# Filler products around the routing's counts, and earlier weight splits in the last expert: a fused attention and mixture-of-experts kernel

## The chip, the cores and the metric

The kernel runs on one core of a Trainium2 chip. The metric is the time of one execution in microseconds (us) on the device. For the kernel before it is 452.43 us, the median of three runs (451.61 to 453.1).

## The reference

Three stages follow each other. A linear attention with a decay per channel runs over 16 (batch, head) pairs of 768 steps, head size 48. Its output, 1536 tokens of 384 numbers, goes through a mixture of 8 experts of which each token takes one, then through a dense layer with a hard-swish.

```python
for t in range(S):
    state = alpha[:, :, t, :, None] * state + np.einsum('bhd,bhe->bhde', k[:, :, t], v[:, :, t])
    y[:, :, t] = np.einsum('bhd,bhde->bhe', q[:, :, t], state)
...
expert_idx = np.argmax(x @ w_gate, axis=1)      # one expert per token, at most 384 tokens each
h = np.maximum(np.einsum('ecd,edf->ecf', disp, w1), 0.0)
y = np.einsum('ecf,efd->ecd', h, w2)            # out[i] = gate_w[i] * y[expert, position]
...
h = x @ w_in
g = h * np.clip(h + 3.0, 0.0, 6.0) / 6.0
out = g @ w_out
```

The model size is 384, an expert's hidden size 1024, the dense layer's 2048.

## The kernel before

The five engines run programs of their own and meet at semaphores.

**Attention** goes over 12 tiles of 128 tokens (NT). TensorE makes scores, state update and output of a tile, turns the output of the tile before (`turn_x`, line 1085) and makes its routing logits (`logits`, line 1093). PSUM has 8 banks, which the stages reuse under other names: `turn_bank` is bank 2, `mix_bank` banks 4 and 5, `y_bank` banks 5 to 7.

**Routing.** VectorE picks each token's expert (`choose`, lines 801 to 809, with the one-hot rows at 805). TensorE turns the one-hot rows into ranks (`ranks_before`, `ranks_within`, lines 1101 to 1112) and, once all tiles are in, into counts per expert (line 1151). This goes in four parts of tiles; the last part, `LATE`, is tiles 10 and 11. GpSimd scatters the gated rows of each token to its slot in DRAM (`slots_x`, line 505), from where SyncE reads an expert's rows back (`load_rows`, line 396). For expert 0 TensorE does not wait for the late tiles' scatter: it gathers their rows with placing matrices that VectorE makes (`place_late`, line 843, products at line 1162), and adds the rows that were read back (line 1167). GpSimd scatters the late tiles only after expert 0's rows are in (`rows_in[0]`), and SyncE reads expert 1's rows (`rows_in[1]`) only after the late scatter is complete.

**Experts.** Weights are used as a sum of two roundings to a shorter float, so each product is three (hi by hi, hi by lo, lo by hi). An expert has 8 hidden tiles f. In step f TensorE makes hidden tile f (lines 1182 to 1184) and the output products of tile f - 3 (lines 1203 to 1205; LAG is 3); the last three tiles' output products of an expert run in the next expert's steps 0 to 2. In steps 3, 4 and 6 (`TURN_AT`) it turns the next expert's rows (`turn_rows`, line 1174), ahead of the first of which it waits for `rows_in`. ScalarE and VectorE follow in the same order: the hidden tile's high part (`hid_hi`, ScalarE, line 662) and rest (`hid_lo`, VectorE, line 946), in step 2 the previous expert's output (`output_hi`, line 653, and `output_lo`, line 926; three chunks c), and the next stage's weight, one of four pieces in each of steps 0, 3, 5 and 7 (`SPLIT_AT`; `split_hi`, line 642, and `split_lo`, line 849). A stage s has four pieces: stages 0 to 7 are the experts, stage 8 (E) is the dense layer's input weight, stage 9 (E + 1) its output weight. SyncE loads a piece into `raw` as soon as VectorE has split the one before it in the same place. In the last expert, pieces of stage 8 are split in steps 0, 3, 5 and 7, and the first piece of stage 9 behind step 7, ahead of the last expert's output.

**Dense layer.** It goes over 4 groups of 384 tokens. Its first products (`first_hidden`, line 1182 again) wait for the last expert's output chunks one by one, and then follow the pattern of the experts with 16 hidden tiles per group.

Of the kernel before, what the change touches and what calls it, by code (L numbers as in the profile page):

```python
# [8 lines left out]
BF16 = mybir.dt.bfloat16  # L9
# [7 lines left out]
def build_program(nc, qk, alpha, v, w_gate, w1, w2, w_in, w_out, out, *, cap):  # L17
    _, D, NT, NPAIR, _ = alpha.shape
    DM = v.shape[2]
    KC = DM // P  # L20
    E = w1.shape[0]
# [21 lines left out]
    FE, FM = F // P, F2 // P  # L43
    PW = KC * 512
    NPC = 4
# [9 lines left out]
    with ExitStack() as ctx:  # L55
        def sb(name, shape, dt=F32):
            return ctx.enter_context(nc.sbuf_tensor(name, shape, dt))

        def sem(name):
            return ctx.enter_context(nc.semaphore(name))  # L60

        bank = [ctx.enter_context(nc.psum_tensor(f"bank{n}", [P, 512], F32)) for n in range(8)]
# [35 lines left out]
        def view(cols):  # L98
            a = arena[0]
            arena[0] += cols  # L100
            assert arena[0] <= ARENA
            return base[:, a:a + cols]
# [78 lines left out]
        zrow = view(DM)  # L181
        tri = sb("tri", [P, P], BF16)
        ones = sb("ones", [P, P], BF16)
# [29 lines left out]
        x_copied = sem("x_copied")  # L213
# [43 lines left out]
        hidden_done = sem("hidden_done")  # L257
# [12 lines left out]
        turn_bank, update_bank = bank[2], bank[3]  # L270
# [2 lines left out]
        xT_bank, logit_bank = bank[6], bank[7]  # L273

        rank_at = [update_bank[:, NPAIR * PR:512]] * 3 + [bank[0][:, :]]
        count_bank = bank[2]
        hidden_bank = bank[0:4]
        rows_bank = bank[4]
        y_bank = bank[5:8]

        TURN_AT = (3, 4, 6)
        SPLIT_AT = (0, 3, 5, 7)
        free_bank = [rows_bank, y_bank[1], y_bank[2]]

        def heads(ap, j):
# [250 lines left out]
        def _(act):  # L536
# [98 lines left out]
            def split_hi(s, w, n):  # L635
                if not isinstance(s, int) or s >= 2:
                    if n < 2:
                        act.wait_ge(hidden_done, (s - 1) * FE)
                    else:
                        act.wait_ge(y_done, (s - 1) * KC)  # L640
                act.wait_ge(raw_in[n], (s + 1) * 16)
                act.activation(w_hi[w][:, n, :], raw[:, n, :], ACT.Copy).then_inc(w_hi_ready, 1)  # L642
# [16 lines left out]
            def expert(e, r):  # L659
                for f in range(FE):  # L660
                    act.wait_ge(hidden_done, e * FE + f + 1)
                    act.activation(hid_hi[f % NH][:, 0:EN], hidden_bank[f % NH][:, 0:EN], ACT.Relu)\  # L662
                        .then_inc(hid_hi_ready, 1)
                    if f == LAG - 1 and not (isinstance(e, int) and e == 0):
                        output_hi(e - 1)
                    if f in TURN_AT and not (isinstance(e, int) and e == E - 1):
                        turn_hi(e + 1, 1 - r, TURN_AT.index(f))
                    if f in SPLIT_AT:
                        split_hi(e + 1, 1 - r, SPLIT_AT.index(f))

            expert(0, 0)
            act.wait_ge(more_end, 1)
            n_more, _ = load_more(act)
# [4 lines left out]
                expert(t * 2 + 1, 1)  # L678
            expert(E - 2, 0)
            expert(E - 1, 1)  # L680
            split_hi(E + 1, 1, 0)
            output_hi(E - 1)

            with act.If(n_more > 0):
# [42 lines left out]
        def _(dve):  # L727
            n = [0]
# [118 lines left out]
            def split_lo(s, w, n):  # L847
                dve.wait_ge(w_hi_ready, s * NPC + n + 1)
                dve.tensor_tensor(w_lo[w][:, n, :], raw[:, n, :], w_hi[w][:, n, :].bitcast(F32), ALU.subtract)\  # L849
                    .then_inc(w_lo_ready, 1)  # L850
# [92 lines left out]
            def expert(e, r):  # L943
                for f in range(FE):
                    dve.wait_ge(hid_hi_ready, e * FE + f + 1)
                    dve.scalar_tensor_tensor(out=hid_lo[f % NH][:, 0:EN], in0=hidden_bank[f % NH][:, 0:EN],  # L946
                                             scalar=0.0, in1=hid_hi[f % NH][:, 0:EN].bitcast(F32),
                                             op0=ALU.max, op1=ALU.subtract).then_inc(hid_lo_ready, 1)
                    if f == LAG - 1 and not (isinstance(e, int) and e == 0):
                        output_lo(e - 1)  # L950
                    if f in TURN_AT and not (isinstance(e, int) and e == E - 1):
                        turn_lo(e + 1, 1 - r, TURN_AT.index(f))
                    if f in SPLIT_AT:
                        split_lo(e + 1, 1 - r, SPLIT_AT.index(f))

            expert(0, 0)
# [5 lines left out]
                expert(t * 2 + 1, 1)  # L962
            expert(E - 2, 0)
            expert(E - 1, 1)
            split_lo(E + 1, 1, 0)
            output_lo(E - 1)

            with dve.If(n_more > 0):
                with dve.Fori(0, n_more) as m:
# [14 lines left out]
                    e = which(m)  # L984
# [42 lines left out]
        def _(pe):  # L1027
# [60 lines left out]
            def logits(i):  # L1088
                pe.wait_ge(xT_copied, i + 1)
                if i >= 1:  # L1090
                    pe.wait_ge(lg_copied, i)
                for c in range(KC):
                    last = pe.matmul(logit_bank[:, i * E:(i + 1) * E], xT[i % 2][:, c * P:(c + 1) * P],
                                     wg[:, c * E:(c + 1) * E], start=(c == 0), stop=(c == KC - 1))
                last.then_inc(logits_done, 1)

            def ranks_before(part):

                a, b = PARTS[part]
                for i in range(a):  # L1100
                    pe.matmul(rank_at[part][:, 0:(b - a) * E].rearrange("p (m e) -> p m e", e=E), ones[:, :],
                              onehot[:, i * E:(i + 1) * E].rearrange("p (o e) -> p o e", o=1)
                              .broadcast_to([P, b - a, E]), start=(i == 0), stop=False, skip_group_check=True)

            def ranks_within(part):
                a, b = PARTS[part]
                pe.wait_ge(onehot_ready, part + 1)
                last = pe.matmul(rank_at[part][:, 0:(b - a) * E], tri[:, :], onehot[:, a * E:b * E], start=(part == 0),
                                 stop=(b - a == 1), skip_group_check=True)
                for i in range(a, b - 1):  # L1110
                    c = i + 1
                    last = pe.matmul(rank_at[part][:, (c - a) * E:(b - a) * E].rearrange("p (m e) -> p m e", e=E), ones[:, :],
                                     onehot[:, i * E:(i + 1) * E].rearrange("p (o e) -> p o e", o=1)
                                     .broadcast_to([P, b - c, E]), start=False, stop=(i == b - 2), skip_group_check=True)
                last.then_inc(ranks_done, 1)
# [30 lines left out]
            pe.wait_ge(masked, NT)  # L1146
            ranks_before(3)
            logits(NT - 1)
            ranks_within(3)
            for i in range(NT):  # L1150
                last = pe.matmul(count_bank[:, 0:E], ones[:, :], onehot[:, i * E:(i + 1) * E],
                                 start=(i == 0), stop=(i == NT - 1))
            last.then_inc(counts_ready, 1)

            def gather_first_rows():

# [54 lines left out]
            n_more, _ = load_more(pe)  # L1211
# [158 lines left out]
```

## Time and profile before

| | us |
|---|---|
| median of three runs | 452.43 (451.61 to 453.1) |
| the profiled execution | 450.51 |
| its span, first to last instruction | 448.0 |
| TensorE products busy in it | 420.9 (94%) |
| VectorE busy | 260.6 (58%) |
| ScalarE busy | 210.8 (47%) |
| GpSimd busy | 53.7 (12%) |
| mean granted clock of TensorE | 0.988 |

Times in the rows are from the span's start. Engines are named PE (TensorE products), PEld (its weight loads), DVE (VectorE), ACT (ScalarE), POOL (GpSimd), SPq (SyncE's DMA issues). The granted clock is a share of 2.4 GHz: 1.00 is that, 0.50 is 1.2 GHz. "L1162" is line 1162. Some products in 32-bit floats have two records each, so a count of x12 can stand for 6 products.

### The profile page before, as it was taken

To read this page: it belongs to the slowest core of one execution; us is meant where nothing else is said; L and a number is where in the kernel's file an instruction comes from. 1 tells how busy PE (TensorE), PEld (TensorE's weight loads), DVE (VectorE), ACT (ScalarE), POOL (GpSimd) and SP (SyncE) were. 2 spreads that over 40 slices of the span, in tenths; PEclk is the share of its full clock that TensorE was granted. 3 is DMA by queue.
4 is the path that set the end of the run, shared out by engine and by line. 5 is a ranking of instruction groups with operands and counts; after the bars stand their busy time and mean duration, and the time that the engine had idled before them with its cause. 6 is when DMAs were issued, how large, how long until landed. Compare 5 with 4: busy or idle time off the path is not lost.

```text
span 448.0 us, 8023 instructions
## 1 busy us (share of the span) xinstructions
PE 420.9 (94%) x3111; PEld 414.6 (93%) x3111; DVE 260.6 (58%) x473; ACT 210.8 (47%) x408; POOL 53.7 (12%) x66
## 2 busy tenths in 40 slices
PE   1899999869999999999998999999999999999993
PEld 1799989859999999999998999999999999999993
DVE  7999999857767767767765563243333333143330
ACT  1254677526565565666663643343334333343331
POOL 9000003630000000000003830110002000110002
PEclk9999999969999999999999999999999999999998
DMA  8999951674856856856758000010001000010001
GB/s 168 284 305 300 311 168 55 183 278 141 255 173 207 251 175 209 246 174 214 222 183 301 4 1 0 15 41 0 1 0 55 0 1 0 4 50 1 0 0 53
DMA packets 37922, 56.34 MB, mean 126 GB/s; under 512 B 4768, under 2 KB 27808, under 8 KB 37888
## 3 DMA queue, kind: packets, MB, share of 16 engines
q1 hardware_dynamic: 35840, 50.95, 37.9%
q0 software_dynamic: 1920, 4.73, 2.7%
q8 instruction: 23, 0.38, 0.4%
q10 hardware_dynamic: 128, 0.20, 0.2%
q14 instruction: 11, 0.09, 0.1%
HBM read 44.06 MB, written 11.81 MB: 125 GB/s over the span
## 4 chain that ended last, share of the span: by engine, by line
PE 86%; DVE 7%; issue 2%; ACT 2%; DMA 1%; POOL 1%; SPq 0%; ACTq 0%; DVEq 0%; POOLq 0%
PE bank L1183 12%; PE bank L1184 12%; PE bank L1182 12%; PE bank L1325 7%; PE bank L1324 7%; PE bank L1323 7%; PE bank L1203 5%; PE bank L1205 5%; PE bank L1204 4%; PE bank L1075 3%; PE bank L1034 2%; PE bank L1053 2%; DVE bwd L744 1%; PE bank L1064 1%; DVE arena L757 1%
## 5 line engine op out<-in xcount | busy, mean ns | idle before, releaser
L849 DVE TENSOR_TENSOR w_lo<-raw,w_hi 128x1536 fp32r<-128x1536 f32 x40 | 70.1, 1758 | 23.3 <-ACT w_hi L642 23.2
L1012 DVE SCALAR_TENSOR_TENSOR arena<-arena,bank 128x384 f32<-128x384 f32 x64 | 35.4, 553 | 82.9 <-ACT arena L713 82.9
L713 ACT ACTIVATE arena<-bank,bias 128x384 f32<-128x384 f32 x64 | 37.0, 577 | 67.9 <-PE bank L1184 67.8
L1182 PE MATMUL bank<-x_hi,w_hi 128*128 128x384 f32 x192 | 64.5, 336 | 1.8 <-DVE w_lo L849 1.8
L1183 PE MATMUL bank<-x_lo,w_hi 128*128 128x384 f32 x192 | 65.1, 339 | 0.0
L1324 PE MATMUL bank<-w_lo,hid_hi 128*128 128x384 f32 x192 | 64.8, 337 | 0.0
L1325 PE MATMUL bank<-w_hi,hid_lo 128*128 128x384 f32 x192 | 64.7, 337 | 0.0
L1184 PE MATMUL bank<-x_hi,w_lo 128*128 128x384 f32 x192 | 64.7, 337 | 0.0
L1323 PE MATMUL bank<-w_hi,hid_hi 128*128 128x384 f32 x192 | 64.6, 337 | 0.0
L1016 DVE SCALAR_TENSOR_TENSOR hid_lo<-arena,hid_hi 128x384 fp32r<-128x384 f32 x64 | 35.7, 558 | 37.9 <-ACT hid_hi L716 37.9
L1182 PE MATMUL bank<-xt_hi,w_hi 128*128 128x232 f32 x192 | 54.4, 283 | 0.1
L716 ACT ACTIVATE hid_hi<-arena 128x384 fp32r<-128x384 f32 x64 | 33.6, 525 | 43.1 <-DVE arena L1012 43.1
L1203 PE MATMUL bank<-hid_hi,w_hi 128*128 128x232 f32 x192 | 53.2, 277 | 0.0
L642 ACT ACTIVATE w_hi<-raw 128x1536 fp32r<-128x1536 f32 x36 | 53.2, 1480 | 0.0
L1205 PE MATMUL bank<-hid_lo,w_hi 128*128 128x232 f32 x192 | 52.9, 275 | 0.0
L1184 PE MATMUL bank<-xt_hi,w_lo 128*128 128x232 f32 x192 | 52.8, 275 | 0.0
L1183 PE MATMUL bank<-xt_lo,w_hi 128*128 128x232 f32 x192 | 52.6, 274 | 0.0
L1204 PE MATMUL bank<-hid_hi,w_lo 128*128 128x232 f32 x192 | 52.5, 274 | 0.0
L662 ACT ACTIVATE hid_hi<-bank 128x232 fp32r<-128x232 f32 x64 | 23.0, 364 | 34.9 <-PE bank L1184 34.9
L1182 PEld LDWEIGHTS bank<-x_hi,w_hi 128*128 128x128 f32 x192 | 36.1, 188 | 1.8 <-DVE w_lo L849 1.8
L1203 PEld LDWEIGHTS bank<-hid_hi,w_hi 128*128 128x128 f32 x192 | 36.8, 192 | 0.5 <-DVE hid_lo L946 0.2
L1182 PEld LDWEIGHTS bank<-xt_hi,w_hi 128*128 128x128 f32 x192 | 36.7, 191 | 0.2 <-issue 0.2
(135 smaller groups left out, 776.8 us busy)
## 6 DMA issues: line engine op xcount, KB each, us to landing
raw<-w SPq DMA_DIRECT2D x32, 768.0 KB, 4.8
slots_x<-arena SPq DMA_DIRECT2D x8, 576.0 KB, 6.6
arena<-qk SPq DMA_DIRECT2D x22, 192.0 KB, 4.7
arena<-slots_x SPq DMA_DIRECT2D x8, 384.0 KB, 4.8
raw<-w_in SPq DMA_DIRECT2D x4, 768.0 KB, 4.3
raw<-w_out SPq DMA_DIRECT2D x4, 768.0 KB, 4.7
arena<-alpha SPq DMA_DIRECT2D x24, 96.0 KB, 4.0
arena<-v SPq DMA_DIRECT2D x12, 192.0 KB, 4.9
```

The lines of the kernel that those rows point to most:

```text
L642: act.activation(w_hi[w][:, n, :], raw[:, n, :], ACT.Copy).then_inc(w_hi_ready, 1)
L713: act.activation(shifted[f % 2], hidden_bank[f % NH][:, 0:BR], ACT.Relu, bias=bias3[:, 0:1]).then_inc(shift_ready, 1)
L849: dve.tensor_tensor(w_lo[w][:, n, :], raw[:, n, :], w_hi[w][:, n, :].bitcast(F32), ALU.subtract)\
L1182: pe.matmul(bank_, hi, hi_in, start=(kc == 0), stop=False)
L1183: pe.matmul(bank_, hi, lo_in, start=False, stop=False)
L1184: return pe.matmul(bank_, lo, hi_in, start=False, stop=(kc == KC - 1))
L1203: pe.matmul(bank_, hi, h_hi, start=(f == 0), stop=False)
L1204: pe.matmul(bank_, lo, h_hi, start=False, stop=False)
L1205: last = pe.matmul(bank_, hi, h_lo, start=False, stop=(f == FE - 1))
L1323: pe.matmul(bank_, h_hi, hi, start=(f == 0), stop=False)
L1324: pe.matmul(bank_, h_hi, lo, start=False, stop=False)
L1325: last = pe.matmul(bank_, h_lo, hi, start=False, stop=(f == FM - 1))
```

## The change

There are two parts.

First, around the last ranks and the counts. A new function `keep_busy(n)` issues n products of the `ones` matrix with 384 columns of `zrow` (zeros, read as bfloat16) into `turn_bank`, whose content nothing reads there any more. Seven go behind the last logits, nine behind the counts. The counts go to bank 5 instead of bank 2, and wait for the last copy of x out of that bank.

Second, in the last expert (E - 1) the pieces of stage 8 are split in steps 0, 1, 3 and 5 and the first piece of stage 9 in step 6; none is left behind the steps. `split_hi` waits, for the first two pieces, for the hidden tiles of the expert that used that piece (4 or 8 of them) and not for all 8 tiles of it or of its successor.

```diff
-        count_bank = bank[2]
+        count_bank = bank[5]
...
+        LAST_SPLIT_AT = (0, 1, 3, 5, 6)
...
             def split_hi(s, w, n):
                 if not isinstance(s, int) or s >= 2:
                     if n < 2:
-                        act.wait_ge(hidden_done, (s - 1) * FE)
+                        act.wait_ge(hidden_done, (s - 2) * FE + 4 * (n + 1))
...
-                    if f in SPLIT_AT:
+                    if isinstance(e, int) and e == E - 1:
+                        if f in LAST_SPLIT_AT[:NPC]:
+                            split_hi(E, 0, LAST_SPLIT_AT.index(f))
+                        elif f in LAST_SPLIT_AT:
+                            split_hi(E + 1, 1, 0)
+                    elif f in SPLIT_AT:
                         split_hi(e + 1, 1 - r, SPLIT_AT.index(f))
...
             expert(E - 1, 1)
-            split_hi(E + 1, 1, 0)
             output_hi(E - 1)
...
+            def keep_busy(n):
+
+                for _ in range(n):
+                    pe.matmul(turn_bank[:, 0:DM], ones[:, :], zrow.bitcast(BF16)[:, 0:DM], start=True, stop=True,
+                              skip_group_check=True)
...
             logits(NT - 1)
+            keep_busy(7)
             ranks_within(3)
+            pe.wait_ge(x_copied, NT)
             for i in range(NT):
                 last = pe.matmul(count_bank[:, 0:E], ones[:, :], onehot[:, i * E:(i + 1) * E],
                                  start=(i == 0), stop=(i == NT - 1))
             last.then_inc(counts_ready, 1)
+            keep_busy(9)
```

VectorE's program has the same edit with `split_lo`.

The order on TensorE from the last tile's turn to the end of expert 0's gather, before:

```order
L1085 MATMUL bank<-ident,x_rows 128x128 x3
L1101 MATMUL bank<-onehot,ones 128x16 x10
L1093 MATMUL bank<-arena 128x8 x3
L1108 MATMUL bank<-onehot,tri 128x16
L1112 MATMUL bank<-onehot,ones 128x8
L1151 MATMUL bank<-onehot,ones 128x8 x12
L1162 MATMUL bank<-arena,x_rows 128x256 x6
L1167 MATMUL bank<-ident,arena 128x128 x6
```

and in the changed kernel, whose line numbers are larger:

```order
L1095 MATMUL bank<-ident,x_rows 128x128 x3
L1117 MATMUL bank<-onehot,ones 128x16 x10
L1103 MATMUL bank<-arena 128x8 x3
L1110 MATMUL bank<-arena,ones 128x384 x7
L1124 MATMUL bank<-onehot,tri 128x16
L1128 MATMUL bank<-onehot,ones 128x8
L1169 MATMUL bank<-onehot,ones 128x8 x12
L1110 MATMUL bank<-arena,ones 128x384 x9
L1181 MATMUL bank<-arena,x_rows 128x256 x6
L1186 MATMUL bank<-ident,arena 128x128 x6
```

The rows of line 1110 are the fillers; nothing else moved.

The order on VectorE in the last expert, from its step 3 to the output of it, before (`w_lo` is a split, `x_lo` an output chunk, `hid_lo` a hidden tile):

```order
L946 SCALAR_TENSOR_TENSOR hid_lo_73<-bank,hid_hi_69 128x232
L849 TENSOR_TENSOR w_lo<-raw,w_hi 128x1536
L946 SCALAR_TENSOR_TENSOR hid_lo_70<-bank,hid_hi_66 128x232
L946 SCALAR_TENSOR_TENSOR hid_lo_71<-bank,hid_hi_67 128x232
L849 TENSOR_TENSOR w_lo<-raw,w_hi 128x1536
L946 SCALAR_TENSOR_TENSOR hid_lo_72<-bank,hid_hi_68 128x232
L946 SCALAR_TENSOR_TENSOR hid_lo_73<-bank,hid_hi_69 128x232
L849 TENSOR_TENSOR w_lo<-raw,w_hi 128x1536 x2
L923 TENSOR_LOAD offsets
```

and in the changed kernel:

```order
L952 SCALAR_TENSOR_TENSOR hid_lo_73<-bank,hid_hi_69 128x232
L855 TENSOR_TENSOR w_lo<-raw,w_hi 128x1536
L952 SCALAR_TENSOR_TENSOR hid_lo_70<-bank,hid_hi_66 128x232
L952 SCALAR_TENSOR_TENSOR hid_lo_71<-bank,hid_hi_67 128x232
L855 TENSOR_TENSOR w_lo<-raw,w_hi 128x1536
L952 SCALAR_TENSOR_TENSOR hid_lo_72<-bank,hid_hi_68 128x232
L855 TENSOR_TENSOR w_lo<-raw,w_hi 128x1536
L952 SCALAR_TENSOR_TENSOR hid_lo_73<-bank,hid_hi_69 128x232
L929 TENSOR_LOAD offsets
```

Two splits stood behind the last hidden tile and ahead of the output; now one stands ahead of the last hidden tile. The other went to step 1, between hidden tiles 1 and 2 and so ahead of expert 6's output chunks:

```order
L952 SCALAR_TENSOR_TENSOR hid_lo_70<-bank,hid_hi_66 128x232
L855 TENSOR_TENSOR w_lo<-raw,w_hi 128x1536
L952 SCALAR_TENSOR_TENSOR hid_lo_71<-bank,hid_hi_67 128x232
L855 TENSOR_TENSOR w_lo<-raw,w_hi 128x1536
L952 SCALAR_TENSOR_TENSOR hid_lo_72<-bank,hid_hi_68 128x232
L929 TENSOR_LOAD offsets
```

The second split of this piece is the one that is new there.

## Rows read from the trace of the kernel before

**Rows 1.** Windows: stretch, length, busy us per engine (instructions), clock, DMA share, GB/s
```profile
92.00:92.67 0.67, 0.00 (x0) 0.00 (x0) 0.39 (x3) 0.17 (x1) 0.13 (x1) 1.00 0.05 18
92.67:95.50 2.83, 0.54 (x14) 0.48 (x15) 2.35 (x15) 1.33 (x3) 0.00 (x0) 0.50 0.29 87
95.50:99.50 4.00, 4.00 (x10) 3.19 (x11) 1.51 (x11) 0.00 (x0) 1.27 (x2) 0.50 1.00 359
99.50:101.50 2.00, 2.00 (x16) 1.88 (x14) 0.31 (x1) 0.62 (x2) 0.68 (x1) 1.00 1.01 378
```

**Rows 2.** Timeline, 91 to 100 us: start, length, engine, line, operation, idle before it
```profile
91.13 0.83 PE L1093 MATMUL bank<-arena 128*128 128x8 f32 x6 [0.34 <-ACT arena L574]
...
93.27 0.20 PE L1108 MATMUL bank<-onehot,tri 128*128 128x16 bf16 x1 [1.30 <-DVE onehot L805]
...
93.34 0.46 PE L1151 MATMUL bank<-onehot,ones 128*128 128x8 bf16 x12
...
95.50 4.81 PE L1162 MATMUL bank<-arena,x_rows 128*128 128x256 f32 x12 [1.70 <-DVE arena L843]
```

**Rows 3.** Timeline of POOL and SPq; then DMA issues around 104 us (KB, us to landing)
```profile
97.93 0.97 POOL L505 DMA_INDIRECT slots_x<-arena,slot  x1 [5.80 <-DMA arena<-slots_x]
...
103.69 0.37 SPq L396 DMA_DIRECT2D arena<-slots_x  x1
...
arena<-slots_x SPq DMA_DIRECT2D x1, 384.0 KB, 3.1
```

**Rows 4.** Timeline of PE in expert 0, steps 3 and 4
```profile
106.83 0.40 PE L1174 MATMUL bank<-ident,arena 128*128 128x128 f32 x2
...
108.25 0.38 PE L1203 MATMUL bank<-hid_hi,w_hi 128*128 128x232 f32 x1
```

**Rows 5.** Timeline of SPq, ACT, DVE and PE around expert 7, steps 0 to 3
```profile
205.00 15.12 SPq L331 DMA_DIRECT2D raw<-w_in  x4
221.77 14.45 SPq L331 DMA_DIRECT2D raw<-w_out  x4
...
218.47 1.49 ACT L642 ACTIVATE w_hi<-raw 128x1536 fp32r<-128x1536 f32 x1
220.22 0.37 ACT L662 ACTIVATE hid_hi<-bank 128x232 fp32r<-128x232 f32 x1 [0.27 <-PE bank L1184]
...
222.89 0.88 ACT L653 ACTIVATE x_hi<-bank 128x232 f32 x3 [0.29 <-PE bank L1205]
...
219.99 1.76 DVE L849 TENSOR_TENSOR w_lo<-raw,w_hi 128x1536 fp32r<-128x1536 f32 x1
...
223.40 1.01 DVE L926 TENSOR_TENSOR x_lo<-bank,x_hi 128x232 f32 x3 [0.37 <-ACT x_hi L653]
...
224.05 0.27 PE L1203 MATMUL bank<-hid_hi,w_hi 128*128 128x232 f32 x1
224.16 0.27 PE L1204 MATMUL bank<-hid_hi,w_lo 128*128 128x232 f32 x1
```

**Rows 6.** Timeline at the hand-over to the dense layer, then its window
```profile
234.07 3.43 DVE L849 TENSOR_TENSOR w_lo<-raw,w_hi 128x1536 fp32r<-128x1536 f32 x2 [0.97 <-ACT w_hi L642]
...
235.74 1.04 ACT L653 ACTIVATE x_hi<-bank 128x232 f32 x3 [0.32 <-PE bank L1205]
...
236.01 0.27 PE L1205 MATMUL bank<-hid_lo,w_hi 128*128 128x232 f32 x1
...
237.42 1.01 DVE L926 TENSOR_TENSOR x_lo<-bank,x_hi 128x232 f32 x3
238.04 0.34 PE L1182 MATMUL bank<-x_hi,w_hi 128*128 128x384 f32 x1 [1.75 <-DVE w_lo L849]
238.21 0.34 PE L1183 MATMUL bank<-x_lo,w_hi 128*128 128x384 f32 x1
...
236.20:238.00 1.80, 0.08 (x1) 0.12 (x1) 1.80 (x3) 0.57 (x2) 0.00 (x0) 1.00 0.46 49
```

**Rows 7.** Instructions of line 926: count, ns min/median/max, first and last start
```profile
L926 DVE TENSOR_TENSOR x_lo<-bank,x_hi x6: 387/392/399, 223.4 to 238.0; 128x232 f32 x6
```

More of the change, by code:

```diff
@@ L952, in expert @@
                         turn_lo(e + 1, 1 - r, TURN_AT.index(f))
-                    if f in SPLIT_AT:
+                    if isinstance(e, int) and e == E - 1:
+                        if f in LAST_SPLIT_AT[:NPC]:
+                            split_lo(E, 0, LAST_SPLIT_AT.index(f))
+                        elif f in LAST_SPLIT_AT:
+                            split_lo(E + 1, 1, 0)
+                    elif f in SPLIT_AT:
                         split_lo(e + 1, 1 - r, SPLIT_AT.index(f))
@@ L964, in _ @@
             expert(E - 1, 1)
-            split_lo(E + 1, 1, 0)
             output_lo(E - 1)
```

## The prediction

> **What bounds the kernel now.** I read the windows first. TensorE is busy through nearly all of the span, so it is the bound, and time can only be won where it waits or runs slowly. Two places stand out. [rows 1] show the first: between 92.67 and 99.5 us the granted clock is 0.50 (1.2 GHz), on both sides of it 1.00 (2.4 GHz). Before it fell the engine had been idle since 91.96 us, and in the half-clock stretch it first had 0.54 us of work in 2.83, then 4.00 in 4.00. The timeline of TensorE [rows 2] shows why: after the last logits it waits 1.30 us for the one-hot rows of the last two tiles, and after the counts 1.70 us for VectorE's placing matrices. The gather (line 1162) then takes 4.81 us, nearly all of it at half clock.
>
> The second place is the hand-over from the experts to the dense layer: TensorE starts the last product of expert 7 at 236.01 us and the first dense product at 238.04, with 1.75 us idle between them [rows 6]. VectorE has been in two weight splits since 234.07, and the three output splits that TensorE waits for (line 926) stand behind them and start at 237.42.
>
> The third view to read is what is late next. [rows 3] follow the late tiles through DRAM: GpSimd scatters them from 97.93 us on, as soon as the first rows have landed, SyncE issues the read of expert 1's rows at 103.69, and that read takes 3.1 us to land, so it is there at about 106.79. The first product that needs it is the transpose at 106.83 [rows 4]. TensorE's arrival and the landing now coincide, with no slack worth naming.
>
> **Part 1, the fillers.** 7 products go between the logits and the last ranks, 9 behind the counts. No row has a bfloat16 product of 384 columns; the nearest is the dense product of as many columns, one starting 0.17 us after the other (238.04, 238.21) [rows 6]. A lower bound for each is the 8-column product: twelve in 0.46 us, 0.04 each [rows 2]; an upper one is 0.34, the same at half clock. I take 0.17 because the columns are the same. Then 7 x 0.17 = 1.19 us, from about 91.9 to 93.1, ahead of the one-hot rows at 93.27; and 9 x 0.17 = 1.53 us from about 93.75 to 95.28, ahead of 95.50. At full clock they fit into the two waits and cost nothing. The counts go to another bank, for which the added wait on the last copy of x has long been met: it is the copy that the transposes ahead already waited for.
>
> If they hold the clock, the 4.00 us between 95.5 and 99.5 [rows 1] become 2.00. The gather (95.50 + 4.81 = 100.31 before) ends 2.0 us sooner, at about 98.3. The first rows are needed there and have landed by 97.93, since GpSimd starts on them then [rows 3]. Everything TensorE does up to the transpose moves from 106.83 to 104.83.
>
> There the gain ends. Nothing in the chain scatter, read, landing waits for TensorE: GpSimd waits for a DMA, SyncE for GpSimd's scatter [rows 3]. TensorE will stand before the transpose from 104.83 until 106.79. Of 2.00 us it keeps 106.83 - 106.79 = 0.04. Behind it the 0.17 us delay at 108.25, where VectorE's rest of hidden tile 1 was late (line 1203) [rows 4], goes too, since VectorE catches up while TensorE stands. The sum for part 1 is 0.04 + 0.17 = 0.2 us. The bounds are 0 and 2.0 us, the second if the landing were as early as TensorE. I take 0.2, by the row of the landing itself.
>
> **Part 2, the splits of expert 7.** The dense layer's input weight is split at steps 0, 1, 3, 5 instead of 0, 3, 5, 7, the first piece of its output weight at step 6 instead of behind step 7. The new waits on hidden tiles ask for 4 or 8 tiles of the expert two stages back, which all steps have long passed; in expert 7 the wait of the output piece falls from 64 tiles done to 60, which step 6 satisfies. The data are there: the four input pieces were issued from 205.00 on over 15.12 us and the first output piece at 221.77 [rows 5], 9 us ahead of step 6 at 230.3. SyncE's later loads and the clearing of the output start some 2 to 4 us sooner; no stall of [rows 6] hangs on them, so I cost that at nothing.
>
> *What it takes away.* ScalarE starts the first output copy at 235.74 [rows 6]. Without splits in between, VectorE follows a start of ScalarE's copy by 0.51 us (222.89 to 223.40) [rows 5], its operation takes 0.39 [rows 7], and TensorE starts 0.23 after its end (237.42 + 0.39 = 237.81, start 238.04) [rows 6]. That makes 235.74 + 0.51 + 0.39 + 0.23 = 236.87 instead of 238.04, a gain of 1.17 us.
>
> *What it adds.* A step is 18 products, 0.112 us apart, so 2.01 us. ScalarE splits at step 1 that much after step 0's split (218.47), right behind the hidden tile of 220.22, so from about 220.48 to 221.97. VectorE's half starts at 221.99 and takes 1.76, so hidden tile 2 comes at 223.66 and the first of expert 6's output splits at 223.97 instead of 223.40 [rows 5]. TensorE's product at 224.05 overwrites the bank that this one reads. Before, 223.40 + 0.39 + 0.23 = 224.02, just in time. Now it is 223.97 + 0.62 = 224.59: TensorE waits 0.54 us, and all of expert 7 behind it moves by as much. The next two chunks are in time, as VectorE's spacing ((1.01 - 0.39) / 2 = 0.31) is below TensorE's three products (3 x 0.11) [rows 5].
>
> *The end of it.* With TensorE 0.54 later the step-6 split runs on VectorE until about 234.3, hidden tile 7 until 234.7, and TensorE wants it at 235.6. The net of part 2 is 1.17 - 0.54 = 0.63 us. The bounds are 1.17 (if the 0.54 does not appear) and 0.3 (if a hidden tile also comes late by as much again as a piece's 0.31).
>
> **Sum.** 0.2 + 0.63 = 0.83 us. The profiled execution took 450.51 us (span 448.0 and 2.5 around it), so it would take 449.7. It was 1.9 us below the median of the runs shown, 452.43; taken from that, 451.6 us. A measurement of this kernel can tell about 0.3%, 1.36 us, from no change: faster means below 451.07, slower above 453.79.
>
> **The rivals.**
> *A, the forecast:* most of the clock's gain is swallowed by the landing of expert 1's rows, 0.83 us remain, 451.6 us. Its own range is 451.0 to 452.1. For it speaks that the chain of [rows 3] never touches TensorE. Chance 0.5.
> *B, the gain gets through:* if the late chain lands by 104.8 in an ordinary execution, TensorE keeps 2.0 + 0.17 us, and with part 2 that is 2.8: 449.6 us. Against it: the issue alone is at 103.69 [rows 3], and it would have to be 2 us earlier. Chance 0.13.
> *C, the other executions lose more to the clock:* the half-clock stretch need not start and end at the same place in each. If the kernel before recovers 1 us later than here, it starts the transpose 0.5 us later, and part 1 is worth 0.7; if 2 us later, 1.2. With part 2 that is 1.3 to 1.8 us, 450.9 us in the middle. That the ordinary runs take 1.9 us more than the profiled one leaves room for this. Chance 0.22.
> The Trainium skill, TensorE: Matmul & The Clock Gate, section on the clock gate, says the monitor runs freely and so the same kernel has more or fewer slow products from run to run. By that rule the gain would differ by execution and C would be the rule rather than the exception; one trace cannot show it.
> *D, the fillers do not hold the clock:* the work ahead of 91.96 is sparse too, and the fillers stream zeros. If the clock still falls at 92.67 and recovers at 99.5, the second group takes 9 x 0.34 = 3.1 us from about 94.0 to 97.1, the gather starts 1.6 us late, and by 99.5 it has had 2.4 us at half clock, worth 1.2. Of its 2.0 + 0.81 = 2.81 us at full clock 1.6 remain, so it ends at 101.1 instead of 100.31, 0.8 lost against 0.63 won: 452.6 us. Chance 0.05.
> *E, the new wait lowers the clock (slower):* TensorE would stand about 2.0 us before the transpose. If the clock falls there as it did at 92.67, it may stay down for the 6.8 us of [rows 1], and dense work loses half of that, 3.4 us: 451.6 + 3.4 = 455.0 us. It decides if an idle time of 2.0 us between dense products is enough. Against it: the 1.75 us at 236.2 left the clock at 1.00 [rows 6]. Chance 0.1.
>
> **How the numbers follow.** Faster is B, C's larger part and A's upper edge: 0.13 + 0.18 + 0.04 = 0.35. Slower is E and a little of D: 0.1. Within 0.3% is the rest, 0.55. The range of 449.6 to 453.0 takes in A, B, C and D and leaves out E and some of B.
>
> **What would show it.** The changed kernel's windows should show the clock at 1.00 from 92 to 98 us, the gather near 2.8 us, and then a new idle time of nearly 2 us before line 1174's counterpart, ended by the DMA of the rows. If that idle time is missing, the part on the landing is wrong. In expert 7 a gap of about 0.5 us before the first output product of step 3 and one of about 0.6 us at the hand-over, in place of 1.75, would confirm part 2. A clock of 0.50 after 106 us would be rival E.

## The result and the profile after

The changed kernel takes 455.05 us (median of 6 runs, 454.51 to 460.91), the kernel before 451.7 beside it (6 runs, 451.18 to 453.1). The ratio is 1.0102, 95% interval 1.007 to 1.0133: slower by about 1%, where the prediction said 451.6 us and 0.2% faster. Ratios here leave out executions that were disturbed from outside, so one can differ a little from the ratio of two medians.

| | before | after |
|---|---|---|
| the profiled execution, us | 450.51 | 454.51 |
| its span, us | 448.0 | 452.7 |
| mean granted clock of TensorE | 0.988 | 0.986 |

I go through the after profile in order of time, the routing first. Timeline of TensorE (line 1110 is the fillers, 1181 the gather, 1193 the transposes), then windows (length, busy of PE, PEld, DVE, ACT, POOL, clock, DMA share, GB/s):

```profile
91.53 1.94 PE L1110 MATMUL bank<-arena,ones 128*128 128x384 bf16 x7
...
93.68 2.48 PE L1110 MATMUL bank<-arena,ones 128*128 128x384 bf16 x9
96.00 2.75 PE L1181 MATMUL bank<-arena,x_rows 128*128 128x256 f32 x12
...
105.57 0.44 PE L1193 MATMUL bank<-ident,arena 128*128 128x128 f32 x2
```
```profile
92.00:94.00 2.00, 2.00 (x22) 1.10 (x20) 1.56 (x12) 0.32 (x2) 0.00 (x0) 0.51 0.29 108
94.00:96.00 2.00, 2.00 (x10) 1.07 (x9) 1.80 (x11) 1.02 (x2) 0.00 (x0) 0.64 0.45 115
96.00:98.00 2.00, 2.00 (x11) 1.77 (x11) 0.80 (x5) 0.00 (x0) 0.21 (x1) 1.00 1.06 398
```

The fillers close both waits of [rows 2]. The clock falls all the same in this execution, from 92.0 us on, but is back at 95.5, ahead of the gather, which takes 2.75 us and not 4.81. The transposes start at 105.57, with no wait ahead of them, because the rows were early too: SyncE issued their read sooner than in [rows 3]:

```profile
102.36 0.37 SPq L398 DMA_DIRECT2D arena<-slots_x  x1
```

So up to here 106.83 - 105.57 = 1.26 us are won, more than the 0.2 of the sum. The delay of 0.17 us at line 1203 [rows 4] mostly went too: the same product starts 1.39 us sooner (106.86 against 108.25). Expert 7's step 0 (hidden tile at 218.77, before 220.22 [rows 5]) is 1.45 us ahead.

Expert 7, in the timelines of ACT, PE and DVE (line 664 is a hidden tile, 655 and 932 are the output splits, 1222 to 1224 the output products, 1201 and 1202 dense products):

```profile
218.77 0.36 ACT L664 ACTIVATE hid_hi<-bank 128x232 fp32r<-128x232 f32 x1 [0.27 <-PE bank L1203]
...
222.48 0.28 PE L1203 MATMUL bank<-xt_hi,w_lo 128*128 128x232 f32 x1
223.07 0.34 PE L1222 MATMUL bank<-hid_hi,w_hi 128*128 128x232 f32 x1 [0.31 <-DVE x_lo L932]
...
234.83 1.04 ACT L655 ACTIVATE x_hi<-bank 128x232 f32 x3 [3.07 <-PE bank L1224]
235.34 1.08 DVE L932 TENSOR_TENSOR x_lo<-bank,x_hi 128x232 f32 x3 [2.12 <-ACT x_hi L655]
...
235.10 0.27 PE L1224 MATMUL bank<-hid_lo,w_hi 128*128 128x232 f32 x1
240.25 0.66 PE L1201 MATMUL bank<-x_hi,w_hi 128*128 128x384 f32 x1 [4.88 <-issue]
240.71 0.52 PE L1202 MATMUL bank<-x_lo,w_hi 128*128 128x384 f32 x1
```

The stall of step 3 is there, ended by the output split as forecast: 0.59 us lie between the starts of two products (222.48 and 223.07) that are otherwise 0.11 apart. And VectorE does what it was freed for: it idles 2.12 us and then follows ScalarE's copy by 0.51 us. But TensorE takes no notice. It starts 4.91 us after the first of these splits (240.25 - 235.34), which last 1.08 us together, and its idle time of 4.88 us is put down to "issue": it waited for no semaphore. The chain of work that ended last goes through the same idle time:

```profile
236.43 3.82 issue
240.25 0.66 PE bank L1201
```

The windows of these microseconds, columns as above, answer to the one of [rows 6]:

```profile
236.00:238.00 2.00, 0.00 (x0) 0.00 (x0) 0.42 (x2) 0.00 (x0) 1.05 (x2) 1.00 1.08 404
238.00:240.00 2.00, 0.00 (x0) 0.00 (x0) 0.00 (x0) 0.00 (x0) 1.70 (x2) 0.70 1.05 391
240.00:242.00 2.00, 1.75 (x6) 1.78 (x7) 0.00 (x0) 0.00 (x0) 1.39 (x3) 0.50 0.49 164
242.00:244.00 2.00, 2.00 (x8) 2.00 (x7) 0.00 (x0) 0.00 (x0) 1.69 (x2) 0.50 0.03 1
244.00:246.00 2.00, 2.00 (x9) 2.00 (x8) 0.00 (x0) 0.00 (x0) 1.40 (x2) 0.59 0.02 1
```

Two things are new against [rows 6]. The clock falls in the gap and stays at 0.50 until about 245.6 us. And the DMA engines, at a share of 0.46 and 49 GB/s in the window of [rows 6], are full (1.08, 404 GB/s). What fills them is the clearing of the output, 2304 KB. SyncE's timeline shows when it is issued, behind the last four weight pieces:

```profile
220.32 10.97 SPq L333 DMA_DIRECT2D raw<-w_out  x4
232.34 0.39 SPq L450 DMA_DIRECT2D out<-arena  x1
```

In the kernel before, SyncE's timeline has it at 237.29 us, by when TensorE was about to start:

```profile
237.29 0.39 SPq L448 DMA_DIRECT2D out<-arena  x1
```

Last, the DMA queues of the changed kernel from 237.6 to 237.7 us, within the gap (queue, kind: packets, MB, share), show a packet of instructions; TensorE resumes at 240.25:

```profile
q1 hardware_dynamic: 25, 0.04, 101.6%
q8 instruction: 1, 0.02, 55.4%
```

**The account.** The span grew by 4.7 us. Expert 7 started 1.45 us earlier and grew by 0.54 (step 0's tile to the last output product: 235.10 - 218.77 = 16.33 us, before 236.01 - 220.22 = 15.79). From that product to the first dense one it is 5.15 us instead of 2.03, +3.12. Behind it the dense products come 0.32 us apart instead of 0.17 for 5.35 us, of which (0.32 - 0.17) / 0.32 is lost, +2.5. The sum is -1.45 + 0.54 + 3.12 + 2.5 = 4.7 us.

### The profile page after: what moved, and what is told of

Read it like the earlier page. It is cut to its first block, busy times and chain, and to the rows that moved or that the text cites. A ratio compares the mean times of both kernels' runs of the same rounds, so it can differ in the third digit from the quotient of the medians.

```text
span 452.7 us, 8059 instructions
## 1 busy us (share of the span) xinstructions
PE 425.1 (94%) x3127; PEld 417.1 (92%) x3127; DVE 260.1 (57%) x473; ACT 210.6 (47%) x408; POOL 48.9 (11%) x66
## 4 chain that ended last, share of the span: by engine, by line
PE 73%; DVE 15%; issue 6%; DMA 4%; ACT 1%; POOL 1%; SPq 0%; DVEq 0%; POOLq 0%; ACTq 0%
PE bank L1203 12%; PE bank L1202 12%; PE bank L1201 12%; PE bank L1344 7%; PE bank L1343 7%; PE bank L1342 7%; PE bank L1222 5%; PE bank L1224 5%; PE bank L1223 5%; DVE bwd L750 3%; DVE arena L779 3%; DVE arena L763 3%; DMA arena<-slots_x 1%; PE bank L1193 1%; DVE arena L795 1%
## 5 line engine op out<-in xcount | busy, mean ns | idle before, releaser
L1201 PE MATMUL bank<-x_hi,w_hi 128*128 128x384 f32 x192 | 65.7, 342 | 4.9 <-issue 4.9
L1202 PE MATMUL bank<-x_lo,w_hi 128*128 128x384 f32 x192 | 66.1, 344 | 0.0
L1203 PE MATMUL bank<-x_hi,w_lo 128*128 128x384 f32 x192 | 65.7, 342 | 0.0
```

Of the source, the lines that this page charges most:

```text
L1201: pe.matmul(bank_, hi, hi_in, start=(kc == 0), stop=False)
L1202: pe.matmul(bank_, hi, lo_in, start=False, stop=False)
L1203: return pe.matmul(bank_, lo, hi_in, start=False, stop=(kc == KC - 1))
```

## The experiments

**Theory 1:** the early splits let SyncE issue the clearing 5 us sooner. Between the last output product and the first dense one TensorE jumps over a block of code for overflowing experts (`n_more > 0`), which this input never runs, and must read the instructions behind it through the same DMA engines. Behind the clearing that read takes long. Two rivals stand against it: the order of the splits, that is the computation itself, and the routing's fillers. The expectations number these differently, so each says what its theory 2 or 3 is; theory 1 is the same in all. Every result is against the kernel before on the same chip (451.48, 451.64, 452.07 and 452.29 us in the four groups of runs).

### Each part alone

`fillers_only` is part 1 of the diff on the kernel before, `splits_only` part 2.

> Only part 1, the filler products and the counts' bank; the splits of the last expert as before. Theory 1 (the loss is the clearing of the output, which part 2 issues 5 us earlier and which then holds up TensorE's instruction reads at the hand-over): part 1 is innocent, the time is that of before or 0.2 to 1.5 us below it, and the first dense product comes about 1.75 us after the last expert product, as before. Theory 2 (the fillers do the harm, by running at half clock ahead of the gather or by moving the clock's later state): this kernel has at least half of the loss of 3.35 us, so 453.4 us or more where before has 451.7.

> Only part 2, the earlier splits of the last expert; no fillers. Theory 1: the whole loss is here. The gap at the hand-over is 4 to 5 us, released by nothing that the profile shows, the clock falls behind it, and the time is 4 to 5 us above before (455.5 to 457), more than the full change's 3.35, since part 1's gain is missing. Theory 2: the time is within 1 us of before, or 0.6 below it as the prediction had it.

Measured: the fillers alone 453.82 us (12 runs), ratio 1.0054 (1.0026 to 1.0082). The splits alone 456.26 us (6 runs), ratio 1.011 (1.0074 to 1.0145). Both are slower, so theory 1 is right on the splits and was wrong to call the fillers innocent. The splits have the gap, here in TensorE's and SyncE's timelines:

```profile
237.25 0.27 PE L1221 MATMUL bank<-hid_lo,w_hi 128*128 128x232 f32 x1
242.52 0.48 PE L1198 MATMUL bank<-x_hi,w_hi 128*128 128x384 f32 x1 [5.00 <-issue]
```
```profile
234.50 0.39 SPq L450 DMA_DIRECT2D out<-arena  x1
```

The fillers alone lose first in another place. Their timeline of TensorE, then windows of the routing, around the transposes and around the first dense product:

```profile
92.28 1.30 PE L1100 MATMUL bank<-arena,ones 128*128 128x384 bf16 x7
...
94.09 1.62 PE L1100 MATMUL bank<-arena,ones 128*128 128x384 bf16 x9
...
108.53 0.69 PE L1183 MATMUL bank<-ident,arena 128*128 128x128 f32 x2 [3.05 <-DMA arena<-slots_x]
```
```profile
94.00:96.00 2.00, 1.75 (x20) 0.94 (x16) 1.75 (x10) 1.13 (x3) 0.00 (x0) 1.00 0.05 20
...
105.40:108.58 3.18, 0.13 (x2) 0.06 (x1) 1.88 (x4) 0.00 (x0) 0.00 (x0) 0.96 0.52 142
108.58:112.00 3.42, 3.42 (x18) 3.42 (x19) 1.38 (x2) 2.10 (x3) 0.00 (x0) 0.54 0.58 217
...
241.34:244.80 3.46, 3.46 (x11) 3.46 (x12) 0.05 (x1) 0.00 (x0) 0.15 (x1) 0.51 1.06 395
```

This is rival E's mechanism. The fillers hold the clock at 1.00, TensorE arrives early, waits 3.05 us for expert 1's rows (issued only at 105.46 us in this execution), and the clock falls behind the wait. It is not the whole loss: this profile also has 2.09 us of idle time ahead of the first dense product and half clock behind it (the last window), where that of the kernel before has 1.75 us and full clock. In the profile of the changed kernel the clock did not hold through the fillers, and the wait for the rows did not come about; so what part 1 is worth depends on when the late chain of [rows 3] lands, and its issue differed by 3.1 us between these two executions (102.36 to 105.46).

### The clearing, moved without any splits

The kernel before with one DMA moved: the clearing ahead of the last weight piece.

```diff
-            load_stage(E + 1)
+            for n, src in enumerate(split_source(E + 1)):
+                if n == NPC - 1:
+                    sp.dma_start(out..., zrow...).then_inc(out_cleared, 16)
+                load_piece(sp, E + 1, n, src)
...
-            sp.dma_start(out..., zrow...).then_inc(out_cleared, 16)
```

> The kernel before, splits untouched, with one line moved: SyncE issues the clearing of the output ahead of the last piece of the output weight, so at about 232 us instead of 237.3. Theory 1: although no product, split or wait of the compute engines has changed, the gap at the hand-over grows from 1.75 us to about 3 to 5 us and the clock falls behind it; the time is 2 to 6 us above before. Theory 3 (the gap comes from the earlier splits or from TensorE reaching the branch sooner, whatever the DMA does): the gap stays at 1.75 us and the time is within 0.5 us of before.

Measured: 455.01 us (6 runs), ratio 1.0083 (1.0066 to 1.0101). TensorE's timeline, the last product of expert 7 and the first dense one, and SyncE's:

```profile
237.32 0.27 PE L1207 MATMUL bank<-hid_lo,w_hi 128*128 128x232 f32 x1
242.40 0.48 PE L1184 MATMUL bank<-x_hi,w_hi 128*128 128x384 f32 x1 [4.81 <-issue]
```
```profile
233.55 0.51 SPq L430 DMA_DIRECT2D out<-arena  x1
```

No computing instruction moved, and yet the gap, the half clock behind it and most of the loss are there. The order of the splits falls as the cause.

The other way round, the clearing held back until the dense layer's third hidden tile, in the changed kernel and in the one before:

```diff
+            sp.wait_ge(hidden_done, E * FE + LAG)
             sp.dma_start(out...).then_inc(out_cleared, 16)
```

> The full change, with one wait added: SyncE issues the clearing of the output only when TensorE has finished the first three hidden tiles of the dense layer. Theory 1: the hand-over gap shrinks to 0.6 to 0.9 us, the clock stays at 1.00 there, and the time is 1.3 to 2.3 us below before (449.4 to 450.4), about 5 us below the full change. Theory 3: the gap stays near 4.9 us and the time at 455.

> The kernel before with the one added wait on the clearing of the output, nothing else. Theory 1: the clearing came only after TensorE's instruction reads in the kernel before too (237.29 us against 235.7), so nothing is gained: within 0.7 us of before. If the clearing still cost something in some executions, up to 1 us faster. Slower by over 1 us would mean that the wait itself hurts the end, where GpSimd's last stores need the cleared output.

Measured: after 452.55 us (12 runs), ratio 1.0019 (0.999 to 1.0047); before 452.03 (10 runs), 1.0021 (0.9998 to 1.0044). One wait takes back most of the loss of the changed kernel and helps the one before not at all. The 449.4 to 450.4 us of the first expectation were missed, though. So was the gap of 0.6 to 0.9 us in it: the profile, of the slowest of the 12 runs, has 2.17 us there, put down to "issue".

### Without the jump

The overflow block taken out of the programs of all engines, in the changed kernel (the clearing still early, at 233.22 us) and in the one before. So the other engines lose their jumps with it, and not TensorE alone. What is left out is the work for experts with more tokens than fit, of which this input has none.

```diff
-            with pe.If(n_more > 0):
-                ...
```

> The full change without the blocks for experts with more than 232 tokens, on all engines (they are skipped with these inputs, so nothing that runs is left out; an input with a fuller expert would lose that part). What goes is TensorE's jump over that code between the last expert product and the first dense one; the clearing of the output stays early. Theory 1a (the gap of 4.9 us is TensorE's fetch of instructions behind that jump, which waits behind the clearing's packets): the gap falls to about 0.9 us although the clearing is as early, the clock stays at 1.00 there, and the time is 3 to 5 us below the full change, 450 to 452. Theory 1b (the clearing holds up something else, or the fetch is needed whether or not there is a jump): the gap stays over 3 us and the time at 454 to 456.

> The kernel before without the overflow blocks (skipped code, as in the other run without them). Its gap is set by VectorE's two splits, not by the jump: 1.75 to 2.0 us as before, and the time within 0.7 us of before. If the jump had cost something in the kernel before as well, the gap would fall below 1.5 us and the time by 0.5 us or more.

Measured: after 450.21 us (10 runs), ratio 0.9973 (0.9949 to 0.9997); before 450.25 (10 runs), 0.998 (0.9952 to 1.0008). The second is 1.8 us below the kernel before beside it (452.07), where at most 0.7 was expected, but the interval of its ratio takes in 1. Timeline of PE and DVE and window of the changed kernel without the block:

```profile
236.17 0.27 PE L1150 MATMUL bank<-hid_lo,w_hi 128*128 128x232 f32 x1
236.91 0.41 PE L1127 MATMUL bank<-x_hi,w_hi 128*128 128x384 f32 x1 [0.47 <-issue]
...
236.41 1.08 DVE L898 TENSOR_TENSOR x_lo<-bank,x_hi 128x232 f32 x3 [2.12 <-ACT x_hi L639]
```
```profile
236.00:238.00 2.00, 1.53 (x10) 1.37 (x10) 1.08 (x3) 0.94 (x3) 0.00 (x0) 1.00 1.06 401
```

The DMA engines are as full as in the changed kernel (1.06, 401 GB/s), yet the gap is 0.47 us. So it is not the store alone, nor any data that the first product needs: it takes store and jump together. No packet of instructions passes between 232 and 241 us. In the kernel before, the gap without the block is still 1.63 us and ends with VectorE's split, so in its profile the jump cost about 0.12 us (1.75 - 1.63):

```profile
237.79 0.41 PE L1108 MATMUL bank<-x_hi,w_hi 128*128 128x384 f32 x1 [1.63 <-DVE w_lo L815]
```

The two kernels without the block are a comparison of the change by itself, with the early clearing made harmless. They take 450.21 and 450.25 us, at ratios of 0.9973 and 0.998 to the kernel before, each on its own chip: even here no gain of the size of the forecast 0.83 us (0.2%) can be told from none.

### Mending both parts

The wait behind the fillers goes when expert 0's steps turn expert 1's rows one step later:

```diff
+        FIRST_TURN_AT = (4, 5, 6)
+
+        def turn_at(e):
+            return FIRST_TURN_AT if isinstance(e, int) and e == 0 else TURN_AT
```

`fillers_late_turn` is part 1 with this; `after_both` is the whole change with this and the held-back clearing.

> Only part 1 (fillers), and in expert 0 the three transposes of expert 1's rows go to steps 4, 5, 6 instead of 3, 4, 6, on all three engines. In the fillers alone the clock held at 1.00 through the gather, TensorE then stood about 3 us before the first of these transposes, for the rows' DMA, and the clock fell to half behind it. Theory A (this wait and the clock behind it ate the gain): with one step of 2 us more ahead of the wait it is 1 us or less, the clock stays at 1.00, and the time is 1.5 to 3 us below the fillers alone, so 450.0 to 452.3 against 451.5 for before. Theory B (the fillers cost time in another way): the time stays at 453.8, the wait shorter or not.

> The full change, with the clearing of the output held until TensorE has made the first three dense hidden tiles, and expert 0's transposes at steps 4, 5, 6. If theories 1 and A are both right, both stalls with their clock falls are gone and this beats the kernel before: 448.9 to 450.5 us against 451.5. If only theory 1 is right, it is at the 452.5 us of the late clearing alone.

Measured: fillers with late turns 452.11 us (12 runs), ratio 0.9974 (0.9943 to 1.0005), as theory A had it. In its profile no idle time stands ahead of the transposes, and the clock is 1.00 until the hand-over. Ten of its runs fall in two groups, 448.7 to 450.2 us at a mean clock of 0.997 to 0.998, and 452.1 to 453.2 at 0.989 to 0.992; the other two took 459.5 at 0.970 and 0.973. All of it together 452.08 us (12 runs), ratio 1.0014 (0.9988 to 1.0039), which misses the 448.9 to 450.5 us that both theories together gave. Timeline and windows of the latter at the hand-over:

```profile
235.77 0.27 PE L1230 MATMUL bank<-hid_lo,w_hi 128*128 128x232 f32 x1
238.00 0.41 PE L1207 MATMUL bank<-x_hi,w_hi 128*128 128x384 f32 x1 [1.96 <-DVE x_lo L938]
...
236.01 1.08 DVE L938 TENSOR_TENSOR x_lo<-bank,x_hi 128x232 f32 x3 [2.12 <-ACT x_hi L661]
```
```profile
236.00:238.00 2.00, 0.04 (x1) 0.03 (x1) 1.08 (x3) 0.54 (x2) 0.67 (x1) 1.00 0.02 4
238.00:240.00 2.00, 2.00 (x8) 2.00 (x9) 0.00 (x0) 0.00 (x0) 1.39 (x3) 0.66 0.05 13
240.00:242.00 2.00, 2.00 (x8) 2.00 (x7) 0.00 (x0) 0.00 (x0) 1.70 (x2) 0.50 0.02 1
```

With the DMA engines empty (0.02) and no split in the way, the gap is still 1.96 us. The profile names `x_lo` as its end, but that stood ready earlier: its first operation started at 236.01 and lasts 0.39 [rows 7], and 236.40 + 0.23 = 236.63 us is when TensorE could have begun. I take the jump for what sets the 1.96 us (the packets below bear this out); then earlier splits win next to nothing at this place, whatever is done about the store. And the clock falls behind this gap too. It need not: in the profile of `late_clear_before` the gap is 1.95 us and the clock stays at 1.00.

Last, 11 more filler products behind the last expert's output products, ahead of the jump. They are already in TensorE's queue while it jumps.

```diff
                 outputs(E - 1, g, 1)
+            keep_busy(11, rows_bank)
```

> Fillers with the late transposes of expert 0 (splits as before), and 11 more filler products behind the last expert product, ahead of the jump over the overflow code. In that kernel's profile the hand-over gap was 2.19 us and the clock fell behind it, and its runs fell into two groups, 449 us at a mean clock of 0.997 and 452 at 0.989. Theory C (the clock falls at the hand-over gap in some executions, and products already in TensorE's queue run while its sequencer fetches): the gap shrinks below 0.5 us, nothing is delayed since the fillers end with VectorE's output split, the upper group vanishes, and the median is 448.8 to 449.8. Theory D (the fillers wait with everything else, or delay the jump): the gap moves behind them, and the time is 452 to 454.

> The same 11 products in the kernel with all of the change, the late clearing and the late transposes. There the gap was 1.96 us, one instruction read long. Theory C: gap below 0.5 us, clock kept, 449.0 to 450.2. The first dense product comes no sooner than without fillers, so against the kernel with the old splits nothing is won: the earlier splits are worth nothing as long as the instruction read sets the gap. Theory D: 452 or more.

> The kernel before plus only the 11 filler products behind the last expert's last output products, ahead of the jump. In all kernels so far the gap there was followed by a half clock in some executions and not in others. If the executions of the kernel before that take 452 us and more are those in which the clock falls behind the 1.75 us gap of the hand-over, the fillers take these away and the median falls by 0.5 to 1.0 us, to a ratio of 0.998 or below. If instead the kernel before keeps its clock there (its profile shows 1.00), the ratio is 1.000 within 0.002, and the 0.9974 of the version with both kinds of fillers comes from the routing's fillers and the later transposes. In both cases the idle time ahead of the first dense product falls from 1.75 us to about 0.7, and that product does not start later than 238.1 us, since VectorE's splits still set it.

| kernel | us (12 runs each) | ratio, 95% interval |
|---|---|---|
| fillers, late turns, these 11 | 450.28 | 0.9974 (0.9958 to 0.9989) |
| the whole change, late clearing, late turns, these 11 | 450.97 | 0.9985 (0.9968 to 1.0002) |
| the kernel before and these 11 alone | 452.06 | 0.9997 (0.9972 to 1.0021) |

Timeline of the first, then two of its windows:

```profile
234.68 1.96 PE L1105 MATMUL bank<-arena,ones 128*128 128x384 bf16 x11
237.60 0.41 PE L1196 MATMUL bank<-x_hi,w_hi 128*128 128x384 f32 x1 [0.95 <-DVE x_lo L931]
```
```profile
236.00:238.00 2.00, 1.05 (x6) 0.62 (x5) 0.98 (x4) 0.00 (x0) 0.00 (x0) 1.00 0.86 301
238.00:240.00 2.00, 2.00 (x14) 2.00 (x13) 0.00 (x0) 0.00 (x0) 0.00 (x0) 1.00 1.07 395
```

The first is faster than the kernel before, by 0.26% with an interval clear of 1, and its runs of 452 us and more are gone (449.44 to 451.68). Its expectation was met in part: the median missed the 448.8 to 449.8 us, and the gap is 0.95 us and not below 0.5. The second missed its 449.0 to 450.2 us, and its gap is 0.80. Both profiles keep the clock at 1.00 at the hand-over. The 11 fillers alone do nothing for the kernel before, as the second theory of their expectation said: its clock holds across 1.75 us anyway. That expectation missed one point: the first dense product came 1.56 us after the first output split had started (239.58 against 238.02), not 0.62 [rows 6]. The fillers take 1.96 us and 0.90 us of idle time follow, more in sum than the 2.0 us of the bare jump, so they hide only part of it. The gain of 0.26% therefore needs the routing's fillers with the late turns. The 11 did not enlarge it (0.9974 with and without them); they narrowed the spread. And the clock still falls somewhere in half of these runs: six of the twelve have a mean clock of 0.995 to 0.997, six of 0.990 to 0.992.

**The packets of instructions.** The trace has the time of each. One of 0.02 MB, all on the same queue, passes near the last output product of expert 7 in each of the twelve profiles of kernels with the block, and in neither of those without it. Six of the twelve, in us:

| profile | last output product starts | packet starts | first dense product starts |
|---|---|---|---|
| before | 236.01 | 235.74 | 238.04 |
| the changed kernel | 235.10 | 237.69 | 240.25 |
| `splits_only` | 237.25 | 240.10 | 242.52 |
| `early_clear_before` | 237.32 | 240.07 | 242.40 |
| `after_both` | 235.77 | 235.37 | 238.00 |
| `join_fill_before` | 236.61 | 236.90 | 239.58 |

In all twelve the first dense product starts 2.3 to 2.8 us behind this packet. In the three with the early store the packet starts 2.6 to 2.9 us behind the last output product's start, in the others between 0.4 ahead and 0.3 behind. So the store delays the packet, and the packet sets when TensorE resumes. With the 11 fillers it comes 0.3 us behind that product instead of 0.1 to 0.4 ahead, which is why the first dense product comes no sooner for them. And in the kernel before, the 2.30 us from packet to product are as short as in any profile: the splits and the jump ended at about the same time.

## Why the prediction was wrong

**The step that failed** stands in part 2: "SyncE's later loads and the clearing of the output start some 2 to 4 us sooner; no stall of [rows 6] hangs on them, so I cost that at nothing." That was true of the stalls before and not of those after. The clearing came 4.95 us sooner (232.34 instead of 237.29), and its 2304 KB fell on the jump. Moving it alone gives a ratio of 1.0083, moving it back in the changed kernel leaves 1.0019, and taking the jump away under it leaves 0.9973 (0.998 in the kernel before): both halves of the mechanism are shown. That what waits behind the store is TensorE's read of instructions rests on the packets: they come late with the store, TensorE resumes at the same distance behind them, and they are absent where the block is gone. The trace does not say for which engine a packet is, so this part stays inferred from the times.

**The 1.17 us at the hand-over** assumed that only VectorE held TensorE back. VectorE's part is right: its output split followed ScalarE's copy by the forecast 0.51 us. Without the jump the first dense product came 0.74 us after the last output product (236.17 to 236.91), against the forecast's 236.87 - 236.01 = 0.86; the 0.23 us from a split's end to the product, read from [rows 6], were 0.11 there (236.41 + 0.39 = 236.80, start 236.91). With the jump and no early store the idle time was 1.75 to 2.19 us in all profiles that have no fillers ahead of it, whatever the splits did. The 1.75 us of [rows 6] hid this second limit of the same length, and the term was worth nothing.

**The stall of 0.54 us** was right: the product is 0.48 us late at the place where it was expected (0.59 - 0.11), held by `x_lo`, and expert 7 as a whole grew by 0.54.

**Part 1, 0.2 us.** The fillers did what was forecast in `fillers_only`: 7 took 1.30 and 9 took 1.62 us (forecast 1.19 and 1.53), with the clock at 1.00. In the profile of the changed kernel they ran while the clock was down; it recovered sooner, and the rows came early by 1.3 us, so that 1.26 us were won instead of 0.2. The landing read from a single execution was taken for fixed, and it is not.

**The rivals.** E's 455.0 us agrees with 455.05 by luck. Its mechanism is real (the late turns, which remove that wait, bring `fillers_only` from a ratio of 1.0054 to 0.9974), but what half clock the changed kernel's profile has behind a wait is at the hand-over, behind one that no rival had. Its counter-argument, that 1.75 us had left the clock at 1.00, is no rule: behind 1.95 us the clock held (`late_clear_before`), behind 1.96 it fell (`after_both`). D's first half came about, the clock fell with the fillers running, but it was back at 95.5 us and not 99.5. The Trainium skill, TensorE: Matmul & The Clock Gate, section on the clock gate, on which C drew, says that the same kernel has more or fewer slow products from one run to the next. The runs agree: with the same program, `fillers_late_turn` had mean clocks from 0.989 to 0.998 in its two groups.

**Open.** Why the clock falls at one gap of about 2 us and holds at another of the same length was not settled, and so neither was which executions land in the upper group of `fillers_late_turn`. The other five runs of the changed kernel have no trace; three of them show a mean clock of 0.992 at about 455 us, so their share of gap and clock can differ from this account.

## What to carry to other kernels

When an edit lets a semaphore come earlier, follow every queue that waits on it to its end, and ask of each transfer issued sooner what else needs the DMA engines at its new time; in a program with branches, that includes the instructions of an engine about to jump. An idle time that the profile puts down to one late operand can hide a second limit of nearly the same length, so test the gap with that operand early before counting on it. If a bulk transfer has no reader soon, tie its issue to the work that it may overlap, not to the end of whatever stood ahead of it in its queue.

## What the runs showed of the hardware

- A jump over a block that is not run left TensorE idle for 1.96 us with empty DMA engines (a share of 0.02, `after_both`), 4.8 to 5.0 us behind a store that held them at a share of 1.05 to 1.08 (the changed kernel, `splits_only`, `early_clear_before`), and 0.47 us where there was no jump (`no_overflow_after`). The first product behind the jump started 2.3 to 2.8 us behind the start of a packet of instructions of 0.02 MB, in twelve profiles.
- Products issued ahead of the jump ran while that packet passed: 11 of them (1.96 us) cut the idle time from 2.19 to 0.95 us. The next product did not come sooner for it: it started 1.62 us after the first output split (237.60 against 235.98), without them 1.06 (237.58 against 236.52).
- Products of 384 bfloat16 columns on zeros took 0.18 us each at full clock (9 in 1.62 us) and went with a granted clock of 1.00 through the routing in six of the eight profiles of kernels that had them. In that of the changed kernel it fell at 92.0 us and in that of `late_clear_after` at 98.7, both while the fillers ran. In all six profiles of kernels without them it fell there.
- Behind idle times of 1.96 to 5.0 us between dense products, dense work ran at half clock (0.52 us a product record instead of 0.34) for another 2.8 to 5.4 us. Behind 1.95 us in `late_clear_before` and 1.75 in the kernel before it ran at 1.00.
